# Attention ahead of two Strassen layers on one core: a pair's output split into an even part and an odd part with both tails, and the tail's copies moved to ScalarE

## The chip, the core and the metric

One core of a Trainium2 chip runs the whole program. The metric is the time of one execution on the device in microseconds, median of several runs. Engines: TensorE (PE: matmuls, their weight loads are PEld), VectorE (DVE), ScalarE (ACT), GpSimd (POOL) and SyncE (SP), which here issues all transfers.

## What is computed

```python
def _attn_ref(q, k, v):                 # q, k, v: (4, 8, 576, 64) fp32
    scores = scale * np.matmul(q, k.transpose(0, 1, 3, 2))
    rel = pos[:, None] - pos[None, :]
    bias = slopes[:, None, None] * (-np.abs(rel))[None, :, :]
    mask = (rel >= 0) & (rel < 128)
    scores = np.where(mask, scores + bias[None], -1000000000.0)
    scores = scores - np.max(scores, axis=-1, keepdims=True)
    attn = np.exp(scores)
    attn = attn / (np.sum(attn, axis=-1, keepdims=True) + 1e-09)
    return np.matmul(attn, v)

# then x = heads side by side: (2304, 512), and two layers:
h = x @ w_in                            # (512, 2048)
g = h * (1.0 / (1.0 + np.exp(-1.702 * h)))     # second layer: a clipped square instead
x = g @ w_out                           # (2048, 512)
```

## The kernel before, in words

The kernel has two stages. The first, attention, takes the first 160 us; the second, the two layers as Strassen-like products of split fp32 operands (`multiply`, line 1053), takes the rest. TensorE passes from one to the other in `duo` (line 1133), whose first call still holds the last pair's transposes.

**Attention.** 32 heads are handled as 16 pairs (an even head and an odd one). A head has 576 rows: four blocks of 128 and a tail of 64. A block of queries sees 256 keys. A pair is five steps (`ITEMS`, line 44): step 1 is block 0 of both heads, step 2 blocks 1 and 2 of the even head, step 3 block 3 of both, step 4 blocks 1 and 2 of the odd head, step 0 the tails of both heads in one bank. Their order in a pair is `STEP_ORDER` = 2, 3, 0, 1, 4 (in the first pair 2, 4, 3, 0, 1), so there are 80 steps, and every engine has a loop over m = 0 to 79 and some drain, written out by hand with lags. Write E for the last step of a pair. At m:

- TensorE (line 1164) makes the scores of step m (line 987), then values times probabilities for a group whose last step lies 4 or 5 steps back (`weigh_values`, lines 1015 and 1021), then transposes the probabilities of step m-2 (line 1000), then, at E+6, the four transposes of a pair's output (`transpose_pair`, line 1030) and at E+9 the one of its tail (`transpose_pair_tail`, line 1035). The tail's probabilities are a group with step 1.
- VectorE (line 1634): at E+5 first `write_pair` (line 1562: add 1e-9 to the sums, reciprocal, multiply), then the bias and the maximum of the scores of step m (line 1557; 1551 for the tails), then extra work: rounding of a head four heads on (line 1533, at E+1 and E+3 of the pair two before; called the cast), some sums and splits of weights and of the next stage's operands at single steps (m = 41, 46, 51, 61, 66, 71, 76), and at E+10 `copy_pair_tail` (line 1573, two copies of 64 x 64).
- ScalarE (line 1278): the copy of the transposed probabilities out of PSUM (line 1234), the exponentials of step m (line 1206; 1201 for the tails), and at E+7 `copy_pair` (line 1229).
- GpSimd (line 936): behind each cast the differences of keys and of queries (lines 889 and 893), and in between some work on weights (903, 913) and operands (929).
- SyncE: loads of heads and values, `store_pair` five pairs behind (line 592, waits for `pair_copied` and `pair_tail_copied`).

A pair's output has ten slots of 65 columns (64 and the sum), slot 2 * block + head; slots 0 to 4 are in PSUM bank 5 and 5 to 9 in bank 6. Three score banks, two for transposed probabilities (3 and 7) and one for transposed outputs (2) are the others. The semaphore `pair_written` is waited for by the next pair's first values (step 2) and by `transpose_pair`; `pair_tail_copied` by the next `transpose_pair`; `pair_copied` by `transpose_pair_tail`; `pair_tail_transposed` by the write after the next.

## Time and profile before

| | us |
|---|---|
| median of 3 runs | 870.99 (870.75 to 872.83) |
| the profiled execution, whole | 870.5 |
| its span, first to last instruction | 868.7 |
| granted clock of TensorE, mean | 0.998 of full |
| busy: TensorE / VectorE / ScalarE / GpSimd | 851.5 / 713.5 / 537.4 / 115.2 |

In rows with a time first, the columns are start and duration in microseconds, then engine, line of the kernel, instruction, and out<-in by the program's names; a bracket at the end is the time that the engine stood idle before it and whose end released it. Ends of matmuls are modelled, so that a row's duration can reach a little past the next row's start. In rows over stretches the granted clock (PEclk) is a share of full speed.

### The profile page before, as it was taken

The page shows a single profiled execution, that of the slowest core. Times are in us where ns is not written, and L with a number is a line of the kernel's source. Part 1 is how long each engine was busy: PE and PEld are TensorE (multiplying, and loading weights), DVE is VectorE, ACT ScalarE, POOL GpSimd, SP SyncE. Part 2 cuts the span into 40 slices and gives each one's busy share as a digit, 9 for nine tenths or more (in the row PEclk, how much of TensorE's full clock was granted, in tenths as well). Part 3 has the DMA queues.
Part 4 walks back from the last instruction along what each step waited for, and adds up shares of the span by engine and source line. Part 5 has one row for each costly group of instructions (what it writes and reads, how often), then busy time and mean ns, then how long its engine had stood idle before and what let it go on. Part 6 is the DMA issues. An engine that isn't in the chain of part 4 may idle for free.

```text
span 868.7 us, 15510 instructions
## 1 busy us (share of the span) xinstructions
PE 851.5 (98%) x5746; PEld 845.4 (97%) x5746; DVE 713.5 (82%) x984; ACT 537.4 (62%) x788; POOL 115.2 (13%) x81
## 2 busy tenths in 40 slices
PE   7999999999999999999999999999999999999998
PEld 7999889999999999999999999999999999999998
DVE  7889897577798868677997988898989779889784
ACT  5887778576774545676744555767556467765441
POOL 4787788000000000000000000000000000000000
PEclk9999999999999999999999999999999999999999
DMA  8876951568667265587775664488556643888822
GB/s 191 214 206 186 241 151 67 189 233 307 219 206 278 97 255 192 210 316 252 266 242 219 243 231 161 135 307 295 195 194 220 229 156 146 290 287 303 307 75 73
DMA packets 63241, 186.45 MB, mean 215 GB/s; under 512 B 7488, under 2 KB 14336, under 8 KB 59328
## 3 DMA queue, kind: packets, MB, share of 16 engines
q1 hardware_dynamic: 63168, 185.46, 63.0%
q8 instruction: 47, 0.77, 0.4%
q14 instruction: 26, 0.21, 0.1%
HBM read 113.09 MB, written 72.35 MB: 213 GB/s over the span
## 4 chain that ended last, share of the span: by engine, by line
PE 87%; DVE 6%; POOL 3%; issue 3%; ACT 1%; DVEq 0%; POOLq 0%; ACTq 0%
PE ps L1053 80%; PE ps L1021 3%; PE ps L987 2%; DVE qk_hi L1533 2%; PE ps L1000 1%; DVE probs L1557 1%; POOL qk_hi L893 1%; POOL k_lo L889 1%; DVE wst L1590 1%; PE ps L1030 0%; PE ps L1015 0%; DVE heads_out L1570 0%; DVE w_first L1603 0%; POOL qk_raw L933 0%; POOL wst L903 0%
## 5 line engine op out<-in xcount | busy, mean ns | idle before, releaser
L1053 PE MATMUL ps<-arena,w_first 128*128 128x384 f32 x1764 | 331.5, 336 | 0.9 <-ACT ps L1305 0.8
L1053 PEld LDWEIGHTS ps<-arena,w_first 128*128 128x128 f32 x1764 | 310.7, 188 | 2.4 <-issue 1.7
L1053 PE MATMUL ps<-arena,w_rest 128*128 128x384 f32 x1260 | 240.8, 337 | 0.9 <-ACT ps L1305 0.8
L1053 PEld LDWEIGHTS ps<-arena,w_rest 128*128 128x128 f32 x1260 | 220.1, 188 | 2.0 <-issue 1.7
L1661 DVE TENSOR_TENSOR arena<-raw_first,arena 128x768 fp32r<-128x768 f32 (+1 forms) x114 | 148.8, 1318 | 78.0 <-ACT arena L1272 78.0
L1272 ACT ACTIVATE arena<-raw_first 128x768 fp32r<-128x768 f32 (+1 forms) x120 | 132.0, 1117 | 45.6 <-DVE raw_first L1619 39.1
L1053 PE MATMUL ps<-w_rest,arena 128*128 128x256 f32 x945 | 132.4, 281 | 0.0
L1053 PEld LDWEIGHTS ps<-w_rest,arena 128*128 128x128 f32 x945 | 121.1, 189 | 0.1
L1053 PE MATMUL ps<-w_first,arena 128*128 128x256 f32 x567 | 88.0, 282 | 0.0
L1661 DVE TENSOR_TENSOR arena<-raw_rest,arena 128x1536 fp32r<-128x1536 f32 (+1 forms) x48 | 71.3, 1486 | 11.6 <-ACT arena L1272 11.5
L1053 PEld LDWEIGHTS ps<-w_first,arena 128*128 128x128 f32 x567 | 76.0, 189 | 0.0
L1272 ACT ACTIVATE arena<-raw_rest 128x1536 fp32r<-128x1536 f32 (+1 forms) x48 | 60.9, 1268 | 23.0 <-PE ps L1053 21.0
L1021 PE MATMUL ps<-v_sb,probs_t 128*128 128x65 f32 x448 | 58.0, 271 | 6.6 <-DVE heads_out L1570 6.6
L1206 ACT ACTIVATE probs<-probs,neg_max 128x256 f32<-128x256 f32 (+1 forms) x128 | 54.1, 472 | 15.3 <-DVE neg_max L1557 15.3
L1021 PEld LDWEIGHTS ps<-v_sb,probs_t 128*128 128x128 f32 x448 | 55.9, 193 | 7.9 <-issue 7.9
L1314 ACT ACTIVATE d1s<-ps 128x384 f32<-128x384 f32 (+2 forms) x72 | 35.3, 490 | 39.9 <-PE ps L1053 39.8
L1305 ACT ACTIVATE ps<-ps 128x384 f32<-128x384 f32 (+2 forms) x72 | 34.0, 475 | 31.0 <-PE ps L1053 31.0
L1590 DVE TENSOR_TENSOR wst<-wst 128x256 f32<-128x256 f32 (+1 forms) x93 | 50.5, 543 | 2.9
L1557 DVE CUSTOM_DVE_ANT_0 probs<-ps,bias_sb 128x256 f32<-128x256 f32 (+1 forms) x128 | 44.6, 385 | 8.7 <-PE ps L987 5.7
L987 PE MATMUL ps<-qk_hi 128*128 128x256 f32 x160 | 48.8, 327 | 1.6 <-POOL k_lo L875 1.4
L1234 ACT ACTIVATE probs_t<-ps 128x512 f32<-128x512 f32 x64 | 37.7, 590 | 16.2 <-PE ps L1000 15.7
L889 POOL TENSOR_TENSOR k_lo<-qk_raw,qk_hi 128x576 fp32r<-128x576 f32 x30 | 43.5, 1450 | 25.4 <-DVE qk_hi L1533 25.0
(116 smaller groups left out, 971.8 us busy)
## 6 DMA issues: line engine op xcount, KB each, us to landing
gd<-g SPq DMA_DIRECT2D x24, 1536.0 KB, 6.1
raw_rest<-gd SPq DMA_DIRECT2D x32, 768.0 KB, 5.1
wst<-w_pairs SPq DMA_DIRECT2D x32, 512.0 KB, 6.1
raw_first<-gd SPq DMA_DIRECT2D x16, 768.0 KB, 6.2
yd<-ust SPq DMA_DIRECT2D x6, 1536.0 KB, 6.3
qk_raw<-qkT SPq DMA_DIRECT2D x30, 288.0 KB, 4.4
wd<-ust SPq DMA_DIRECT2D x4, 1536.0 KB, 9.4
raw_first<-yd SPq DMA_DIRECT2D x4, 1536.0 KB, 7.8
```

The costliest lines, as they stand in the source:

```text
L889: nc.gpsimd.tensor_tensor(k_lo[:, slot], keys(qk_raw, head), f32(keys(qk_hi, head)), ALU.subtract).then_inc(qk_split[slot], 1)
L987: last = nc.tensor.matmul(place, queries, k[:, key0:key0 + BAND], start=n_pass == 0 and (d > 0 or i == 0), stop=n_pass == 1 and (d > 0 or ...
L1021: last = nc.tensor.matmul(o_slot(2 * blk + e), probs_t[:, gi % 2, col:col + P], v_sb[:, h + e, max(blk - 1, 0) + piece], start=piece == 0, ...
L1053: last = nc.tensor.matmul(to, stationary, moving, start=start and n == 0, stop=n == len(steps) - 1, skip_group_check=True)
L1206: last = nc.scalar.activation(at, at, ACT.Exp, bias=neg_max[:, col:col + 1], scale=-1.0)
L1234: nc.scalar.activation(probs_t[:, gi % 2], pt_bank[gi % 2], ACT.Copy).then_inc(pt_copied[gi % 2], 1)
L1272: nc.scalar.activation(operand(k, i)[:, 0], source(k, i), ACT.Copy).then_inc(hi_made, 1)
L1305: nc.scalar.activation(b_bank(D, pos), a_bank(D, pos), ACT.Copy).then_inc(seeded_b, 1)
L1314: nc.scalar.activation(d1(D, pos), d_bank(D, pos), ACT.Copy).then_inc(d_copied, 1)
L1557: last = nc.vector.tensor_tensor_reduce(out=to[:, 0:width], in0=bank[:, i * BAND:i * BAND + width], in1=bias_sb[:, h + e, BAND - width:BAN ...
L1590: nc.vector.tensor_tensor(to, a, b, ALU.subtract).then_inc(w_added, 1)
L1661: nc.vector.tensor_tensor(at[:, 1], source(k, i), f32(at[:, 0]), ALU.subtract).then_inc(lo_made, 1)
```

## The change

The ten slots are laid out anew: bank 5 holds blocks 0 to 3 of the even head, bank 6 blocks 0 to 3 of the odd head and then both tails. Each bank is a part with its own write, its own tile of inverses and its own semaphore. VectorE writes the even part at E+4 and the odd part at E+5, each behind the bias of that step (before: both at E+5, ahead of it). The next pair's values wait for the part that they overwrite: step 2 for the even part, step 3 for both. The pair's transposes come at E+7 (before E+6), its copy on ScalarE at E+8 (before E+7). The tail's transpose stays at E+9 and its copies at E+10, but the copies are ScalarE's, save the last pair's.

```diff
+OUT_SLOTS = (((0, 0), (0, 1), (0, 2), (0, 3)), ((1, 0), (1, 1), (1, 2), (1, 3), (0, 4), (1, 4)))
...
-WRITE_LAG = 5
-PAIR_LAG = 6
-COPY_LAG = 7
+WRITE_LAGS = (4, 5)
+PAIR_LAG = 7
+COPY_LAG = 8
 PAIR_TAIL_LAG = 9
 COPY_TAIL_LAG = 10
...
-    o_banks = ps[:, 5:7, 0:SLOTS // 2 * VALUES].rearrange("p b (s n) -> p b s n", n=VALUES)
+    o_banks = [ps[:, bank, 0:slots * VALUES].rearrange("p (s n) -> p s n", n=VALUES)
+               for bank, slots in zip((5, 6), map(len, OUT_SLOTS))]
...
+    def out_part(e, blk):
+        return int((e, blk) not in OUT_SLOTS[0])
+
+    def o_slot(e, blk, count=1):
+        part = out_part(e, blk)
+        slot = OUT_SLOTS[part].index((e, blk))
+        return o_banks[part][:, slot] if count == 1 else o_banks[part][:, slot:slot + count]
...
-                wait_past(pe, pair_written, q)
+            for part in range(2):
+                if any(out_part(e, blk) == part for e, blk in ITEMS[d]):
+                    wait_past(pe, written[part], q)
...
-                    nc.tensor.matmul(o_banks[:, 1, 3:5], probs_t[:, gi % 2, col:col + P],
+                    nc.tensor.matmul(o_slot(0, 4, 2), probs_t[:, gi % 2, col:col + P],
...
-                    last = nc.tensor.matmul(o_slot(2 * blk + e), probs_t[:, gi % 2, col:col + P],
+                    last = nc.tensor.matmul(o_slot(e, blk), probs_t[:, gi % 2, col:col + P],
...
         def transpose_pair(q):
-            pe.wait_ge(pair_written, q + 1)
+            for part in range(2):
+                pe.wait_ge(written[part], q + 1)
...
+        def copy_pair_tail(q):
+            pair = q % BATCH_PAIRS
+            act.wait_ge(pair_tail_transposed, q + 1)
+            for half in range(2):
+                rows = slice(half * TAIL, (half + 1) * TAIL)
+                last = nc.scalar.activation(x_pairs[rows, pair, 4 * P:SEQ], xt_bank[rows, rows], ACT.Copy)
+            last.then_inc(pair_tail_copied, 1)
...
-        for m in range(ALL_STEPS + TRANSPOSE_LAG):
+        for m in range(ALL_STEPS + DRAIN + 1):
...
             if (q := pair_at(m, COPY_LAG)) is not None:
                 copy_pair(q)
+            if (q := pair_at(m, COPY_TAIL_LAG)) is not None:
+                copy_pair_tail(q)
...
-        def write_pair(q):
-            at = inverse[:, q % SUM_RING]
-            dve.wait_ge(pv_done, 4 * (q + 1))
-            nc.vector.tensor_scalar(at, o_banks[:, :, :, DIM], 1e-9, None, ALU.add).then_inc(sums_guarded, 1)
...
+        def write_out(q, part):
+            at, bank = inverse[part][:, q % SUM_RING], o_banks[part]
+            to = heads_out[:, q % 2].rearrange("p (b e d) -> p b e d", e=2, d=DIM)
+            last = max(i for i, (pair, m) in enumerate(GROUPS)
+                       if pair == q and any(out_part(e, blk) == part for e, blk in ITEMS[ORDER[m][1]]))
+            dve.wait_ge(pv_done, last + 1)
+            nc.vector.tensor_scalar(at, bank[:, :, DIM], 1e-9, None, ALU.add).then_inc(sums_guarded, 1)
+            dve.wait_ge(sums_guarded, 2 * q + part + 1)
+            nc.vector.reciprocal(at, at).then_inc(sums_inverted, 1)
+            dve.wait_ge(sums_inverted, 2 * q + part + 1)
             wait_past(dve, pair_tail_transposed, q - 1)
...
+            last = nc.vector.tensor_tensor(to[:, 0:4, part], bank[:, 0:4, 0:DIM],
+                                           at[:, 0:4].unsqueeze(2).to_broadcast([P, 4, DIM]), ALU.mult)
+            if part:
+                last = nc.vector.tensor_tensor(to[:, 4], bank[:, 4:6, 0:DIM],
+                                               at[:, 4:6].unsqueeze(2).to_broadcast([P, 2, DIM]), ALU.mult)
+            last.then_inc(written[part], 1)
...
-            if (q := pair_at(m, WRITE_LAG)) is not None:
-                write_pair(q)
             if m < ALL_STEPS:
                 bias_scores(m)
+            for part in range(2):
+                if (q := pair_at(m, WRITE_LAGS[part])) is not None:
+                    write_out(q, part)
...
-            if (q := pair_at(m, COPY_TAIL_LAG)) is not None:
-                copy_pair_tail(q)
```

## Rows read from the trace of the kernel before

**Rows 1.** The page: busy time, and the chain that ended last, by line.
```profile
PE 851.5 (98%) x5746; PEld 845.4 (97%) x5746; DVE 713.5 (82%) x984; ACT 537.4 (62%) x788; POOL 115.2 (13%) x81
...
PE ps L1053 80%; PE ps L1021 3%; PE ps L987 2%; DVE qk_hi L1533 2%; PE ps L1000 1%; DVE probs L1557 1%; POOL qk_hi L893 1%; POOL k_lo L889 1%; DVE wst L1590 1%; PE ps L1030 0%; PE ps L1015 0%; DVE heads_out L1570 0%; DVE w_first L1603 0%; POOL qk_raw L933 0%; POOL wst L903 0%
```

**Rows 2.** Stretches: length, busy PE, PEld, DVE, ACT, POOL, clock, DMA share, GB/s.
```profile
40.00:60.00 20.00, 20.00 (x183) 20.00 (x182) 17.15 (x65) 15.27 (x37) 16.30 (x12) 1.00 0.75 196
...
120.00:140.00 20.00, 16.95 (x150) 16.61 (x151) 19.77 (x57) 14.18 (x30) 16.49 (x11) 1.00 0.36 101
```

**Rows 3.** Timeline of VectorE, line 1570: four writes of a pair.
```profile
31.40 0.82 DVE L1570 TENSOR_TENSOR heads_out<-ps,inverse 128x640 f32<-128x640 f32 x1
39.46 0.82 DVE L1570 TENSOR_TENSOR heads_out<-ps,inverse 128x640 f32<-128x640 f32 x1
...
72.08 0.82 DVE L1570 TENSOR_TENSOR heads_out<-ps,inverse 128x640 f32<-128x640 f32 x1
...
81.89 0.82 DVE L1570 TENSOR_TENSOR heads_out<-ps,inverse 128x640 f32<-128x640 f32 x1
```

**Rows 4.** Waits, 0 to 170 us: total, times, longest.
```profile
PE ps L1021 <- DVE heads_out L1570: 6.6, 7, 1.5
```

**Rows 5.** Timeline, 74 to 85 us: casts on VectorE, GpSimd's operations beside them.
```profile
74.40 1.83 POOL L913 TENSOR_TENSOR w_first<-wst,w_first 128x768 fp32r<-128x768 f32 x1
...
74.71 2.14 DVE L1533 CAST qk_hi<-qk_raw 128x1152 fp32r<-128x1152 f32 x1
...
78.48 2.01 POOL L893 TENSOR_TENSOR qk_hi<-qk_raw,qk_hi 64x576 fp32r<-64x576 f32 x1
...
79.41 1.69 DVE L1533 CAST qk_hi<-qk_raw 128x1152 fp32r<-128x1152 f32 x1
...
84.99 0.76 DVE L1533 CAST qk_hi<-qk_raw 128x1152 fp32r<-128x1152 f32 x1 [0.41 <-DMA qk_raw<-qkT]
```

**Rows 6.** Timeline of VectorE around the write at 81.89.
```profile
81.24 0.28 DVE L1557 CUSTOM_DVE_ANT_0 probs<-ps,bias_sb 128x128 f32<-128x128 f32 x1
...
81.45 0.15 DVE L1565 TENSOR_SCALAR inverse<-ps 128x10 f32<-128x10 f32 x1
81.64 0.22 DVE L1567 RECIPROCAL inverse<-inverse 128x10 f32<-128x10 f32 x1
...
82.63 0.41 DVE L1557 CUSTOM_DVE_ANT_0 probs<-ps,bias_sb 128x256 f32<-128x256 f32 x1
...
83.31 0.45 DVE L1578 COPY x_pairs<-ps 64x64 f32<-64x64 f32 x2
```

**Rows 7.** The chain that ended last, in order of time, near 50 us: start, length.
```profile
50.25 1.30 DVE qk_hi L1533
```

**Rows 8.** Timeline of TensorE: values behind the wait for a write.
```profile
101.41 1.08 PE L1021 MATMUL ps<-v_sb,probs_t 128*128 128x65 f32 x8 [0.97 <-DVE heads_out L1570]
...
147.57 1.08 PE L1021 MATMUL ps<-v_sb,probs_t 128*128 128x65 f32 x8 [0.21 <-DVE heads_out L1570]
```

**Rows 9.** Timeline at the end of attention, 154 to 157 us.
```profile
154.70 0.17 DVE L1565 TENSOR_SCALAR inverse<-ps 128x10 f32<-128x10 f32 x1 [5.12 <-PE ps L1021]
...
154.84 1.22 PE L1053 MATMUL ps<-arena,w_first 128*128 128x384 f32 x6
...
156.48 0.63 PE L1030 MATMUL ps<-ident,heads_out 128*128 128x128 f32 x4 [0.42 <-DVE x_pairs L1578]
```

**Rows 10.** ScalarE's copies from 30 to 130 us: busy, mean ns, idle before.
```profile
L1229 ACT ACTIVATE x_pairs<-ps 128x512 f32<-128x512 f32 x12 | 7.0, 582 | 0.0
...
L1256 ACT ACTIVATE w_first<-wst 128x256 fp32r<-128x256 f32 x2 | 0.8, 409 | 0.0
```

**Rows 11.** Timeline, 46 to 48 us: exponentials of a tail, then a tail's transpose.
```profile
46.24 0.46 ACT L1201 ACTIVATE probs_tail<-probs_tail,neg_max 128x192 f32<-128x192 f32 x1
...
47.32 0.27 PE L1035 MATMUL ps<-ident,heads_out 128*128 128x128 f32 x1
```

**Rows 12.** Stretches around the low clock, columns as in rows 2.
```profile
98.00:102.00 4.00, 2.61 (x22) 2.23 (x21) 3.93 (x16) 2.83 (x5) 2.54 (x3) 1.00 0.40 105
102.00:106.00 4.00, 4.00 (x24) 4.00 (x24) 2.86 (x11) 2.31 (x6) 3.08 (x4) 0.57 1.03 296
```

More of the change, by code:

```diff
@@ L151, in build @@
     neg_max = sb("neg_max", [P, 2 * (STEPS - 1) + TAIL_RING], F32, attn_ctx)
-    inverse = sb("inverse", [P, SUM_RING, 2, SLOTS // 2], F32, attn_ctx)
+    inverse = [sb(f"inverse{part}", [P, SUM_RING, len(OUT_SLOTS[part])], F32, attn_ctx) for part in range(2)]
     probs_t = sb("probs_t", [P, 2, 4 * P], F32, attn_ctx)
@@ L194, in build @@
     sums_inverted = sem("sums_inverted")
-    pair_written = sem("pair_written")
+    written = [sem("first_part_written"), sem("second_part_written")]
     pair_transposed = sem("pair_transposed")
@@ L317, in all_queries @@
         return tile[rows, head % SPLIT_RING, at:at + SEQ]
-    def o_slot(slot):
-        return o_banks[:, slot // (SLOTS // 2), slot % (SLOTS // 2)]
+    def out_part(e, blk):
[4 more added lines that the diff above has]
+        return o_banks[part][:, slot] if count == 1 else o_banks[part][:, slot:slot + count]
     def up_duo(u, c, dd):
@@ L1560, in bias_scores, with copy_last_tail @@
             last.then_inc(scores_biased, 1)
-        def write_pair(q):
-            at = inverse[:, q % SUM_RING]
-            dve.wait_ge(pv_done, 4 * (q + 1))
-            nc.vector.tensor_scalar(at, o_banks[:, :, :, DIM], 1e-9, None, ALU.add).then_inc(sums_guarded, 1)
-            dve.wait_ge(sums_guarded, q + 1)
+        def write_out(q, part):
[6 more added lines that the diff above has]
+            dve.wait_ge(sums_guarded, 2 * q + part + 1)
             nc.vector.reciprocal(at, at).then_inc(sums_inverted, 1)
-            dve.wait_ge(sums_inverted, q + 1)
+            dve.wait_ge(sums_inverted, 2 * q + part + 1)
             wait_past(dve, pair_tail_transposed, q - 1)
-            nc.vector.tensor_tensor(heads_out[:, q % 2].rearrange("p (b s d) -> p b s d", b=2, d=DIM), o_banks[:, :, :, 0:DIM],
-                                    at.unsqueeze(3).to_broadcast([P, 2, SLOTS // 2, DIM]), ALU.mult).then_inc(pair_written, 1)
-        def copy_pair_tail(q):
-            pair = q % BATCH_PAIRS
-            dve.wait_ge(pair_tail_transposed, q + 1)
+            last = nc.vector.tensor_tensor(to[:, 0:4, part], bank[:, 0:4, 0:DIM],
[4 more added lines that the diff above has]
+            last.then_inc(written[part], 1)
+        def copy_last_tail():
+            dve.wait_ge(pair_tail_transposed, PAIR_COUNT)
             for half in range(2):
                 rows = slice(half * TAIL, (half + 1) * TAIL)
-                last = nc.vector.tensor_copy(x_pairs[rows, pair, 4 * P:SEQ], xt_bank[rows, rows])
+                last = nc.vector.tensor_copy(x_pairs[rows, BATCH_PAIRS - 1, 4 * P:SEQ], xt_bank[rows, rows])
             last.then_inc(pair_tail_copied, 1)
@@ L1633, in _ @@
         round_first(0)
-        for m in range(ALL_STEPS + COPY_TAIL_LAG - 1):
-            if (q := pair_at(m, WRITE_LAG)) is not None:
-                write_pair(q)
+        for m in range(ALL_STEPS + WRITE_LAGS[1]):
             if m < ALL_STEPS:
                 bias_scores(m)
+            for part in range(2):
+                if (q := pair_at(m, WRITE_LAGS[part])) is not None:
+                    write_out(q, part)
             if m == 0:
@@ L1779, in up @@
                 if k == 0:
-                    copy_pair_tail(PAIR_COUNT - 1)
+                    copy_last_tail()
                 add_weights(w + (3 if u < 2 else 4))
```

## The prediction

> **What bounds the kernel now.** I read the page first: TensorE is busy 98% of the span, and line 1053, the product stage, makes up 80% of the chain that ended last [rows 1]. The diff touches only the attention stage, the first 160 us. So the question is how much earlier attention can end; from there on TensorE runs without a gap, and what attention saves the whole keeps.
>
> Inside attention the stretches come next [rows 2]. From 40 to 60 us TensorE is busy throughout and VectorE 17.15 of 20; from 120 to 140 VectorE is busy 19.77 and TensorE 16.95. The engine that sets the pace changes. The starts of the write of a pair show the same [rows 3]: 8.06 us from 31.40 to 39.46, but 9.81 from 72.08 to the next write at 81.89 [rows 3]. Of the fifteen distances between the sixteen writes four are slow like this one; a fifth slow one has another cause, below. The waits then name what the change aims at: TensorE waits 6.6 us in seven places for the write of a pair (L1570 before L1021) [rows 4]. That 6.6 is the naive gain.
>
> It isn't the gain that I expect, since waiting is where TensorE's slack shows in a slow pair, not what makes it slow. VectorE's own rows in the pair before 81.89 have no gap: a cast of 2.14 us at 74.71, then an extra operation on weights, then a cast of 1.69 at 79.41 [rows 5]. Casts take 0.76 where GpSimd is quiet (84.99). The long ones end about 0.6 us after GpSimd's operation beside them: 74.40 + 1.83 = 76.23 against 76.85, and 78.48 + 2.01 = 80.49 against 81.10 [rows 5]. GpSimd in turn waits for the cast. The slow pair is thus a loop of cast, GpSimd, extra operation, cast; the write lies behind the second cast and outside the loop. The Trainium skill (SBUF — State Buffer, "SBUF: two separate sides") says that VectorE in a two-port mode and GpSimd exclude each other for a whole instruction; by that rule the cast's length is a wait that swallows work put ahead of it. These rows agree. By the rule VectorE's extra work there (0.10 a pair, below) costs nothing; by the bare durations it would cost 0.5 over five pairs.
>
> **The change, part by part.**
>
> Work on VectorE. A pair costs it now, from start to start: sum 0.19 (81.45 to 81.64), reciprocal 0.25 (to 81.89), multiply 0.74 (from 81.89 to 82.63) [rows 3, 6], and two tail copies, 0.45 busy together [rows 6], 0.48 with the hand-over: 1.66. After: sum and reciprocal twice, 0.88 (their small widths matter little: I keep the price for 10 columns), and multiplies of 256, 256 and 128 columns. The 640-column one takes 0.74 to the next start. If its columns cost 1.04 ns each, as 0.82 busy less a fixed 0.15 (the 10-column sum's whole duration) says, it has 0.67 of columns and 0.07 fixed, so 0.34 + 0.34 + 0.20 = 0.88. Sum 1.76, or 0.10 more a pair; between 0 (narrow sums are cheaper) and 0.3 (each of four extra instructions costs its own 0.15 without overlap, less the copies). In the loop above it is hidden by GpSimd; in fast pairs by VectorE's gaps of 1.2 to 1.7 us. It shows only where GpSimd is back to back, in the 16 us of the chain behind the cast at 50.25 [rows 7]. That cast starts after both parts instead of after write and copies: later by about 0.15. **Cost 0.15.**
>
> The earlier release. The next pair's first values (step 2) now need only the first part, which is behind one score operation and 0.78 us of writing instead of 1.18: 0.40 sooner, so I take 0.46 with the shorter end of the multiply. But step 3 needs the second part: 0.78 + 0.76 (bias of the next step: 0.68 from 82.63 to 83.31, and hand-over) + 0.98 + 0.1 of hand-over = 2.6 after the last short bias (begun at 81.24, over at 81.45) [rows 6], that is 84.1; TensorE's own path, led by 0.46, gets there at about 84.1 too. Net lead 0.36, between 0.2 and 0.46. It counts only where a slow pair is followed by a TensorE-bound one: from the values at 101.41 on, and again a pair before 147.57 [rows 8]. **Gain 0.72.** In other slow pairs the wait only moves. At 147.57 TensorE waits 0.21 by the row [rows 8]; modelled ends run some 0.16 past the next start, so really about 0.37. Even part written by then: **gain 0.37.**
>
> The end. At 156.48 the last pair's transposes waited (0.42 by the row) for the tail copy of the pair before, queued behind the last write; the product ahead of them began at 154.84 and needs 1.22 less the modelled 0.16, to 155.90 [rows 9]. Now ScalarE copies that tail from about 154.8, where its queue is empty, and the last odd part is ready at 154.70 + 0.19 + 0.25 + 0.34 + 0.25 + 0.1 = 155.83, before the transposes can start at 155.95. **Gain 0.53** (between 0.3 and 0.6).
>
> Tail copies on ScalarE. No row shows it copying 64 columns. Below: half of VectorE's 0.45 for two [rows 6]; above: its own 256-column copy of 0.41. I take 0.28 each, by 0.58 for 512 columns and the slope between those two [rows 10]. The Trainium skill (VectorE: DVE Perf Modes, "The TRN2 errata") gives ScalarE 172 + columns cycles from PSUM, which would be an estimate of 0.20; nothing would change. About 0.5 a pair, where ScalarE is busy 15.27 of 20 us [rows 2]: hidden. The transposes of a pair (lag 7) need this copy (lag 10 of the pair before, the same step less two): it ends about 42.4, they run at about 43.8. Slack 1.4.
>
> The pair copy one step later (lag 8). It now comes after the tail's exponentials at 46.24 and starts 0.36 behind them, at 46.60, ending 47.18; TensorE loads the tail's transpose 0.11 before 47.32 [rows 11]. With 0.05 of hand-over it is late by about 0.04 where it had slack of over a microsecond. Eight TensorE-bound pairs: **cost 0.30**, bounds 0 and 1.6 (0.2 each). In slow pairs this wait is larger (the copy would end near 80.6, the tail's transpose was due at about 79.9), but TensorE has 1.5 us to spare there and merely waits earlier.
>
> SyncE stores a pair five pairs later than the one being loaded; that leaves a tail about 10 us. No DMA is added or moved, and half a microsecond more on a tail doesn't reach its queue.
>
> Sum: 0.72 + 0.37 + 0.53 - 0.15 - 0.30 = **1.17 gained** against the profiled execution's 870.5. The runs' median is 870.99, so I forecast 869.8.
>
> **Rivals.** (A) *The clock stays up.* The granted clock is 0.57 on average from 102 to 106, once in attention [rows 12]: mostly the lower level, 1.2 of 2.4 GHz. It follows four microseconds in which TensorE was busy 2.61. Lost: 4 x 0.43 = 1.7, which makes the fifth slow pair. In the other slow pairs the idle is one block and the clock held. After the change much idle moves ahead of the tail's transpose, as one block of some 1.6. For: the idle is short and can go either way. Against: the busy total of four microseconds hardly changes. 869.8 - 1.7 = 868.1.
> (B) *The waits were the bound*: all 6.6 and the 0.42 at the end go, and the clock's 1.7: 871.0 - 8.7 = 862.3. Against it is VectorE without a gap.
> (C) *Slower: the pair copy.* If ScalarE reaches it later than worked out (the exponentials of the tail, weights rounded and tail copies in the same queue), the tail's transpose holds every score behind it. At 0.3 us in each of 16 pairs it costs 4.8 in place of 0.3: 874.3. It decides from (2.6 + 1.17 + 0.3) / 16 = 0.25 a pair. For it: the slack I work out is nothing. Against: ScalarE has idle stretches in every pair.
> (D) *VectorE's additions count*: the casts don't absorb them in the five slow pairs (0.5), and the lead of 0.72 is lost: 869.8 + 1.2 = 871.0. The ends of the casts speak against.
>
> **How the numbers follow.** Forecast 0.38, A 0.30, B 0.08, C 0.10, D 0.14. A measurement can tell about 0.3% from no change, 2.6 us. Faster than 868.4: A lies 0.3 beyond that line, so most of it, and all of B, with a part of the forecast's own scatter, 0.32. Slower than 873.6: C and a little more, 0.10. Within: 0.58. The range leaves out B and C: from 867.2 (A with costs at 0 and gains at their upper ends is 867.4, and runs scatter by some tenths) to 871.6 (D, with the pair copy at 0.11 a pair).
>
> **What would show it.** Right: VectorE's rows without a gap and write-to-write distances near 9.8 in the same slow pairs; the wait of L1021 for a write well under 6.6, with a new wait of TensorE at the tail's transpose (L1035) for ScalarE's pair copy in its place; the last pair's transposes directly behind the product. Wrong: slow pairs near 8.1 (B), a wait at L1035 in pairs that took 8.06 (C), or 8.06 itself changed. A low clock anywhere in attention tells A from the forecast.

## The result, and the profile after

The changed kernel takes **872.4 us**, median of 20 runs (871.99 to 874.97), beside 870.92 of the kernel before, also 20 runs (870.5 to 872.83). The ratio is 1.0015, 95% interval 1.0009 to 1.0021: slower by 1.5 us, less than 0.2% but clear of no change, where the prediction had 1.17 us of gain and a range that ended at 871.6. The profiled execution took 872.12 us, its span 870.3.

First the page of the changed kernel: busy time, and the chain that ended last, by line. The product stage is now line 1066, the scores 997, the values 1033, the transposes of a pair 1043, the cast 1556, GpSimd's two differences 899 and 903.

```profile
PE 853.2 (98%) x5746; PEld 843.8 (97%) x5746; DVE 713.7 (82%) x1018; ACT 544.9 (63%) x818; POOL 114.3 (13%) x81
...
PE ps L1066 80%; PE ps L1033 3%; PE ps L997 2%; PE ps L1010 2%; DVE qk_hi L1556 2%; POOL qk_hi L903 2%; POOL k_lo L899 1%; DMA qk_raw<-qkT 1%; PE ps L1043 1%; DVE probs L1580 1%; PE ps L1027 1%; DVE wst L1620 0%; ACT w_first L1280 0%; SPq L583 0%; SPq L582 0%
```

The totals hardly move against [rows 1]: VectorE has 0.2 us more. The busy totals don't tell where 1.5 us went. One name is new in the chain: a load of heads (DMA qk_raw<-qkT, 1%), which [rows 1] doesn't have. The same stretches as in [rows 2] and [rows 12] (length, busy PE, PEld, DVE, ACT, POOL, clock, DMA share, GB/s) tell more:

```profile
40.00:60.00 20.00, 19.64 (x173) 19.01 (x172) 16.68 (x69) 15.95 (x40) 15.63 (x12) 1.00 0.73 198
...
120.00:140.00 20.00, 17.90 (x151) 16.59 (x150) 19.73 (x61) 15.50 (x36) 16.38 (x11) 1.00 0.38 101
...
98.00:102.00 4.00, 3.10 (x29) 2.86 (x27) 3.96 (x8) 2.20 (x5) 2.63 (x2) 1.00 0.79 199
102.00:106.00 4.00, 3.52 (x29) 3.28 (x30) 3.64 (x20) 3.96 (x10) 3.56 (x3) 1.00 0.54 166
```

From 40 to 60 us TensorE, which had no gap before, starts 173 matmul instructions instead of 183: the pairs that TensorE used to pace are now slower. And the clock stays at its upper level, 2.4 GHz, from 102 to 106. Rival A's condition came true, and the time still rose.

The start of the tail's transpose (L1035 before, L1048 after) marks each pair. The distances between these sixteen starts, in us, worked out from the timelines:

```
          first at  pairs up to 82             then one, four, one, one  last two   last at
before      31.19   8.05 8.08 8.08 8.07 8.40 8.05   9.78 | 8.67 11.50 8.05 8.81 | 9.84 9.81 | 8.12 5.02   159.52
after       31.66   8.11 8.51 8.31 8.50 8.51 8.50   9.47 | 10.73 8.56 8.51 9.82 | 9.83 9.48 | 7.76 4.80   161.06
difference  +0.47   +1.71 in all                   -0.31 | +0.59 in all         | -0.01 -0.33 | -0.36 -0.22  +1.54
```

The sum, 1.54, is the whole loss. The largest part is 1.71 in the six pairs that TensorE used to pace: four now take 8.50 instead of 8.05 to 8.40. The +0.47 at the start is not read further: over all kernels of this document that first start lies anywhere from 30.9 to 31.8. The middle four hold, before, the low clock; more on that below.

The load lies just ahead of the distance of 10.73. In the chain of waits (start, length) it releases the cast of an even head at 87.28:

```profile
81.71 5.54 DMA qk_raw<-qkT
```

The waits of the changed kernel from 0 to 172 us (total, times, longest):

```profile
POOL k_lo L899 <- DVE qk_hi L1556: 28.0, 27, 2.5
...
PE ps L997 <- POOL qk_hi L903: 3.2, 9, 0.5
...
PE ps L1033 <- DVE heads_out L1597: 1.9, 5, 0.4
PE ps L1048 <- ACT x_pairs L1242: 1.7, 4, 1.2
```

TensorE's wait for a write fell from 6.6 [rows 4] to 1.9, as the change meant it to. But 3.2 us of waiting for GpSimd and 1.7 for ScalarE's pair copy stand there now: 6.8 in all, so the waits have changed their name. And the same view of the kernel before gives GpSimd less idleness:

```profile
POOL k_lo L889 <- DVE qk_hi L1533: 25.0, 25, 1.9
```

GpSimd waits 3 us longer for casts after the change. The chain of waits of the changed kernel, in order of time (start, length), shows where GpSimd stands in the path. It is one full turn of a pair, in the fourth of the six distances, from the scores at 53.24 to those at 61.74, and the turn is 8.50 us long:

```profile
53.24 0.49 PE ps L997 x4
...
53.93 0.11 DVE probs_tail L1574
...
54.30 1.90 DVE qk_hi L1556
...
56.33 1.43 POOL k_lo L899
...
57.83 1.41 POOL qk_hi L903
...
59.29 0.74 PE ps L997 x4
60.03 0.84 PE ps L1033 x8
60.86 0.44 PE ps L1010 x4
61.31 0.44 PE ps L1043 x4
61.74 0.47 PE ps L997 x4
```

Read it as a loop: scores of the tails (step E+8, which is E+3 of the next pair), their bias, the cast of the odd head, GpSimd's two differences, and then the scores of E+7, which need the head just split, with their values and transposes, until the scores of E+8 again. Of this turn GpSimd's stretch is fixed. What TensorE does between the scores of E+7 and those of E+8 is not covered by anything. The change has put the four transposes of the pair there (L1043, 0.44). Not every slow turn is this loop: in the fifth distance the chain runs from 63.52 to 67.45 through ScalarE's queue, its copy of the pair (0.39) among it.

A second part is in VectorE. This is its timeline in the changed kernel, from the bias of E+5 to the casts, with GpSimd's operations beside them:

```profile
48.28 0.27 PE L1048 MATMUL ps<-ident,heads_out 128*128 128x128 f32 x1
...
49.26 0.43 DVE L1580 CUSTOM_DVE_ANT_0 probs<-ps,bias_sb 128x256 f32<-128x256 f32 x1 [0.62 <-PE ps L1010]
...
50.10 0.16 DVE L1592 TENSOR_SCALAR inverse<-ps 128x6 f32<-128x6 f32 x1
...
51.05 0.41 DVE L1580 CUSTOM_DVE_ANT_0 probs<-ps,bias_sb 128x256 f32<-128x256 f32 x1
...
51.74 0.77 DVE L1556 CAST qk_hi<-qk_raw 128x1152 fp32r<-128x1152 f32 x1
...
52.65 1.42 POOL L899 TENSOR_TENSOR k_lo<-qk_raw,qk_hi 128x576 fp32r<-128x576 f32 x1 [0.76 <-DVE qk_hi L1556]
...
54.15 1.42 POOL L903 TENSOR_TENSOR qk_hi<-qk_raw,qk_hi 64x576 fp32r<-64x576 f32 x1
...
54.22 1.97 DVE L1556 CAST qk_hi<-qk_raw 128x1152 fp32r<-128x1152 f32 x1
```

The odd cast, 1.97 us long, ends at 56.19, 0.62 behind the end of GpSimd's operation at 54.15 + 1.42 = 55.57, as the long casts of [rows 5] did. Before, the whole write stood ahead of the bias of E+5 and began while VectorE still waited for these scores, so it was free; behind the bias only the tail's copies stood (0.48). After, the odd part stands behind that bias: 50.10 to 51.05, 0.95. From the tail's transpose to the even cast it was 50.17 - 47.32 = 2.85 before and is 51.74 - 48.28 = 3.46 here; in all six pairs the cast starts 0.45 to 0.6 later than it did.

Whether GpSimd then starts later is another question, and in this pair it doesn't. These are the same two operations in the kernel before:

```profile
50.17 1.38 DVE L1533 CAST qk_hi<-qk_raw 128x1152 fp32r<-128x1152 f32 x1
...
51.69 1.42 POOL L889 TENSOR_TENSOR k_lo<-qk_raw,qk_hi 128x576 fp32r<-128x576 f32 x1 [0.76 <-DVE qk_hi L1533]
```

The cast came earlier but ran longer, until 51.55, 0.62 behind the end of GpSimd's work on weights (50.93), and GpSimd's difference began 51.69 - 47.32 = 4.37 behind the tail's transpose; after, 52.65 - 48.28 = 4.37. The timelines of the other pairs show that the late cast reaches GpSimd only in the first two of the six (4.16 against 3.71 in both); in the last four GpSimd's work on weights covers it. What is late in the pair shown is the odd cast, by 0.24, because the values of E+7 wait for the odd part (1.04 in the chain for 0.84) and the tails' scores come behind them. TensorE waits for GpSimd where the late cast reaches it, at 42.46, and again at 59.29:

```profile
42.46 0.39 PE L997 MATMUL ps<-qk_hi 128*128 128x256 f32 x1 [0.17 <-POOL qk_hi L903]
...
59.29 0.39 PE L997 MATMUL ps<-qk_hi 128*128 128x256 f32 x1 [0.19 <-POOL qk_hi L903]
...
61.50 0.37 PE L997 MATMUL ps<-qk_hi 128*128 128x256 f32 x1
```

At the same place before, GpSimd's operation ended at 56.62 + 1.41 = 58.03, just ahead of the scores that need it at 58.10, and from these to the next scores it was 1.77 us against 61.50 - 59.29 = 2.21:

```profile
57.75 0.60 PE L1030 MATMUL ps<-ident,heads_out 128*128 128x128 f32 x4
...
58.10 0.37 PE L987 MATMUL ps<-qk_hi 128*128 128x256 f32 x1
...
59.87 0.37 PE L987 MATMUL ps<-qk_hi 128*128 128x256 f32 x1
```

From this came two theories, which can both hold: **late transposes** (L in the expectations below: the pair's transposes at E+7 lie in the uncovered part of the loop) and **late cast** (W: the odd part stands ahead of the even cast, and GpSimd starts late). Their rivals were the prediction's C (ScalarE's pair copy at the tail's transpose) and D (VectorE's additional work by its mere amount).

### The profile page after: what moved, and what is told of

Its sections match the earlier page's. It is cut to its first block, busy times and chain, and to the rows that moved or that the text cites. A ratio compares the mean times of both kernels' runs of the same rounds, so it can differ in the third digit from the quotient of the medians.

```text
span 870.3 us, 15634 instructions
## 1 busy us (share of the span) xinstructions
PE 853.2 (98%) x5746; PEld 843.8 (97%) x5746; DVE 713.7 (82%) x1018; ACT 544.9 (63%) x818; POOL 114.3 (13%) x81
## 4 chain that ended last, share of the span: by engine, by line
PE 88%; DVE 4%; POOL 3%; issue 2%; DMA 1%; ACT 1%; SPq 1%; DVEq 0%; POOLq 0%; ACTq 0%
PE ps L1066 80%; PE ps L1033 3%; PE ps L997 2%; PE ps L1010 2%; DVE qk_hi L1556 2%; POOL qk_hi L903 2%; POOL k_lo L899 1%; DMA qk_raw<-qkT 1%; PE ps L1043 1%; DVE probs L1580 1%; PE ps L1027 1%; DVE wst L1620 0%; ACT w_first L1280 0%; SPq L583 0%; SPq L582 0%
## 5 line engine op out<-in xcount | busy, mean ns | idle before, releaser
L1328 ACT ACTIVATE ps<-ps 128x384 f32<-128x384 f32 (+2 forms) x72 | 34.0, 475 | 28.8 <-PE ps L1066 28.8
```

The source lines that it names most:

```text
L1328: nc.scalar.activation(b_bank(D, pos), a_bank(D, pos), ACT.Copy).then_inc(seeded_b, 1)
```

## The experiments

Thirteen kernels ran. Each ratio is against the kernel before, on the same chip. "After" and "before" in front of an edit say which kernel it was made in.

**e1_pair8** (after): the pair's transposes one step later still, out of that part of the loop.

```diff
-PAIR_LAG = 7
+PAIR_LAG = 8
```

> The changed kernel with the pair's transposes one step later still (lag 8 instead of 7). Theory L (loop): in the fast pairs the scores of the odd head (step E+7) wait for GpSimd's split of that head, which follows the cast behind the tail's bias (scores of E+3); the change put the pair's transposes (0.44 us) between the scores of E+7 and those of E+8, the one stretch of that loop in which GpSimd has nothing to do. At lag 8 they lie under GpSimd's work again: fast pairs go back from 8.50 to about 8.1, some 2.2 us less up to 82 us, whole time 869 to 870.3. Rival W (VectorE): the second write in front of the even cast makes the loop long by itself; the distances stay at 8.5 and the time at 872.4. Rival C (ScalarE's pair copy at the tail's transpose): stays at 872.4 or gets worse, since the copy is closer to the tail's transpose.

Measured: 871.84, ratio 1.0005 [0.9996, 1.0014], above what was expected. The 0.5 us that it gains is no larger than the uncertainty of the two medians. Its first distances are 8.12 8.22 8.31 8.21 8.69 8.41, not 8.06, so something else holds the loop as well.

**e2_before_pair7** (before): only the transposes and their copy one step later, with one whole write as before.

```diff
-PAIR_LAG = 6
-COPY_LAG = 7
+PAIR_LAG = 7
+COPY_LAG = 8
...
-        for m in range(ALL_STEPS + TRANSPOSE_LAG):
+        for m in range(ALL_STEPS + TRANSPOSE_LAG + 1):
```

> The kernel before with only the pair's transposes one step later (lags 7 and 8 for 6 and 7). Theory L by itself: up to 0.44 us more in each TensorE-bound pair, less where GpSimd's split is done early (from 44.65 to 49.54 in the trace of before, 0.5 ahead of its scores): between 871 and 873.5. If theory W holds alone, no change: 870.9. Theory C (copy one step later behind the tail's exponentials): waits at the tail's transpose in the fast pairs, 0.04 to 0.3 each.

Measured: 871.7, ratio 1.0010 [1.0001, 1.0019], 0.8 us slower. Its distances are 8.06 8.11 8.06 8.51 8.52 8.48, then 9.48 9.85 8.57 8.48 9.82 9.82 9.5, 8.1, 5.03. The fourth to sixth are those of the changed kernel to 0.02, so the 8.50 there comes from this move alone. The first three are not (8.06 8.11 8.06 against 8.11 8.51 8.31): these 0.7 us, and more in the middle (9.85 against 10.73), belong to the rest of the change. The run moves ScalarE's copy of the pair together with the transposes, and doesn't tell the two apart. Ahead of the 9.85 the load is shorter: 5.2 us from its issue to the cast that waits for it, against 6.1 in the changed kernel, and that cast starts 1.4 us earlier. It has the wait of the tail's transpose for ScalarE's pair copy too, in five places against four (here and in the experiments below, fences of this form are waits from 0 to 172 us):

```profile
PE ps L1021 <- DVE heads_out L1570: 3.6, 5, 0.8
...
PE ps L1035 <- ACT x_pairs L1229: 1.8, 5, 1.2
```

**e3_pair6** (after): transposes and copy where they were before.

```diff
-PAIR_LAG = 7
-COPY_LAG = 8
+PAIR_LAG = 6
+COPY_LAG = 7
```

> The changed kernel with the transposes back at lag 6 and the copy at 7. They then need the odd part, which VectorE finishes about 0.6 us after TensorE gets there. Theory L: the wait takes the place of the 0.44, fast pairs 8.5 to 8.7, time 872 to 873.5, and no wait of the scores for GpSimd. Theory C: the pair copy is early again, so 870 to 871.

Measured: 875.39, ratio 1.0054 [1.0041, 1.0067]. Far slower, for a reason that I hadn't expected. The transposes don't wait for the odd part but for ScalarE's copies of the tail of the pair before, in 14 pairs:

```profile
PE ps L1043 <- ACT x_pairs L1249: 10.7, 14, 1.2
```

The first eight distances are 8.87 to 9.08. So the transposes *had* to move once the copies had become ScalarE's.

**f3_before_act_tails** (before): nothing but the tail's copies moved to ScalarE (`copy_pair_tail` as in the diff, at E+10 behind `copy_pair`), to ask that directly.

> The kernel before with only the tails' copies moved to ScalarE (all but the last pair's), lags as they were. The transposes of the next pair at E+6 then wait for a copy that stands behind the exponentials of E+5 (with lag 6 in the changed kernel that wait was 10.7 us in 14 places, 0.6 to 1.2 each). Expected: waits of 0.5 to 0.7 in each pair, fast pairs 8.6 to 8.9, 873 to 876. If ScalarE's copies are hidden as the prediction had it, 870.5.

Measured: 874.14, ratio 1.0036 [1.0023, 1.0048], with the same wait:

```profile
PE ps L1030 <- ACT x_pairs L1236: 9.4, 14, 0.8
```

The copies themselves are short, but ScalarE reaches them too late for transposes at E+6.

**f4_dve_tails** (after): the tail's copies back on VectorE, behind the odd part (`copy_last_tail(q)` at COPY_TAIL_LAG for every pair).

> The changed kernel with the tails' copies back on VectorE behind its other work of the step (two parts and lag 7 stay). Theories L and W: 0.48 us more in front of the even cast in each pair, so the loop over GpSimd is longer still: fast pairs 8.6 to 9.0, 873.5 to 876, and the last pair's transposes wait again for the copy. If VectorE's work in front of the cast is free: 872.4.

Measured: 873.22, ratio 1.0027 [1.0018, 1.0036], 0.8 slower than the changed kernel, with intervals that just touch. The six fast distances are 0.7 longer in all, and GpSimd's first difference starts later in each of them, by 0.26 to 0.49. This is the direct measure of what 0.48 us more ahead of the even cast costs. With the new write order ScalarE's copies do pay; they take 0.48 out of what lies between bias and cast.

**e4_half_split** (after): GpSimd's difference for the queries made for 288 columns of 576. This leaves out the low part of half of the queries.

```diff
-                nc.gpsimd.tensor_tensor(all_queries(qk_hi, head, LOWER), all_queries(qk_raw, head, UPPER),
-                                        f32(all_queries(qk_hi, head, UPPER)), ALU.subtract).then_inc(qk_split[slot], 1)
+                nc.gpsimd.tensor_tensor(all_queries(qk_hi, head, LOWER)[:, 0:SEQ // 2], all_queries(qk_raw, head, UPPER)[:, 0:SEQ // 2],
+                                        f32(all_queries(qk_hi, head, UPPER)[:, 0:SEQ // 2]), ALU.subtract).then_inc(qk_split[slot], 1)
```

> The changed kernel with GpSimd's difference of the queries made for 288 of the 576 columns only (left out: the low part of half of the queries of most heads). Each such operation is about 0.7 us shorter. Theories L and W, both of which need GpSimd in the chain: fast pairs back to 8.1, slow pairs shorter by 1 or more, time 866 to 869. Theory C or a chain of TensorE, VectorE and ScalarE alone: fast pairs stay at 8.5.

Measured: 863.34, ratio 0.9912 [0.9898, 0.9926]. Nine microseconds go, more than expected, and the first six distances are 8.11 to 8.33. The two rows are groups of instructions from 30 to 130 us (busy, mean ns | idle before), the first of the changed kernel, the second of this one:

```profile
L903 POOL TENSOR_TENSOR qk_hi<-qk_raw,qk_hi 64x576 fp32r<-64x576 f32 x23 | 35.1, 1526 | 1.8
```

```profile
L903 POOL TENSOR_TENSOR qk_hi<-qk_raw,qk_hi 64x288 fp32r<-64x288 f32 x24 | 21.9, 913 | 1.9
```

0.61 us less per head, 1.2 per pair. The slow pairs fall from 9.5 to 9.8 to between 8.2 and 9.0, and TensorE's wait for GpSimd's queries is gone from the list. VectorE has the same instructions in this kernel, but its casts are shorter as well, 1.045 us in the mean against 1.344, since they end behind GpSimd's operations. This puts GpSimd into the path. It speaks against D, though VectorE's busy time fell too, so it doesn't exclude it.

**g1_cast1** (after): the even cast one step earlier, so that it stands ahead of the odd part.

```diff
-CAST_LAG = (2, 3)
+CAST_LAG = (1, 3)
```

> The changed kernel with the even head's cast one step earlier, transposes at lag 7 as in the change. With the runs so far (changed 872.4, lag 8 alone 871.8, lag 8 and early cast 870.2) this closes the square. If the two effects add, 872.4 - 1.6 = 870.8. If the place of the transposes costs 0.44 by itself whenever GpSimd's second split ends late, fast pairs stay at 8.3 to 8.5 in part: 871 to 872. If only the cast's lateness mattered: 870.2, as with lag 8.

Measured: 870.58, ratio 0.9994 [0.9985, 1.0003]. The second distance is back at 8.12, the first six together are 50.36 against 50.44, and the sixth alone is longer, 9.05.

**f1_pair8_cast1** (after): both, `PAIR_LAG = 8` and `CAST_LAG = (1, 3)`.

> The changed kernel with the pair's transposes at lag 8 and the cast of the even head one step earlier on VectorE (lag 1 for 2), so ahead of the bias of step E+6. In the first run with lag 8 the fast pairs took 8.2 to 8.7, not 8.06. Theory W (the second write in front of the even cast makes GpSimd's split of the even head end late, and the odd cast wait for it): the cast ahead gives that back, fast pairs 8.06 to 8.1, no wait of the scores for GpSimd before 80 us; 870.5 or less, against 871.8 with lag 8 alone. If the lateness of the even cast does not matter, 871.8 again.

Measured: 870.18, ratio 0.9992 [0.9983, 1.0001]. With e1 and g1 this is a square, of medians with intervals about 0.8 us to each side:

```
                         transposes at E+7     at E+8
even cast at lag 2            872.4 (after)      871.8 (e1)
even cast at lag 1            870.6 (g1)         870.2 (f1)
```

In time alone, the early cast gives 1.7 (1.8 and 1.6 with either place of the transposes), clear of the intervals; the transposes' place gives 0.5 (0.6 and 0.4), which isn't. But the 1.7 is what a whole step earlier gives, and not what the change's half microsecond had cost. The fast pairs gain next to nothing (f1: 8.12 8.11 8.31 8.22 8.42 9.04, where 8.06 to 8.1 was expected); from the seventh tail's transpose to the last it is 78.96 in the changed kernel and 77.75 in g1, so the gain lies in the slow pairs. The load that the cast at 87 waits for also differs: from issue to cast 6.1 us in the changed kernel, 6.6 in e1, 6.5 in g1 and 5.4 in f1, one execution of each, so part of the difference between e1 and f1 may be its scatter.

**f2_before_cast1** (before): `CAST_LAG = (1, 3)` alone, to see if it is simply a better place.

> The kernel before with only the cast of the even head one step earlier. Theory: GpSimd's idle time ahead of its splits (25.0 us before) falls wherever it sets the pace, so the slow pairs shorten or the stretch behind 48 us loses its 0.4; 869.5 to 870.9. The rival, that VectorE's total alone counts: 870.9.

Measured: 882.94, ratio 1.0135 [1.0121, 1.0149]. Twelve microseconds slower: in the old order the cast came to stand ahead of the tail's copies, for which the transposes wait:

```profile
PE ps L1030 <- DVE x_pairs L1578: 14.3, 13, 2.0
```

**g2_before_cast1_copy** (before): the same, with the tail's copies moved ahead of the cast.

```diff
-CAST_LAG = (2, 3)
+CAST_LAG = (1, 3)
...
+            if (q := pair_at(m, COPY_TAIL_LAG)) is not None:
+                copy_pair_tail(q)
...
-            if (q := pair_at(m, COPY_TAIL_LAG)) is not None:
-                copy_pair_tail(q)
```

> The kernel before with the even cast one step earlier but behind the tail's copies (in the run with the cast ahead of them TensorE waited 13.9 us for those copies, 882.9). Theory: fast pairs are TensorE's own 8.06 and stay; slow pairs, which are the loop of cast and GpSimd, get GpSimd's start some 0.7 earlier and shorten from 9.8 towards 9.1: 868.5 to 870. The rival, that in the slow pairs VectorE's busy time is the bound: 870.9.

Measured: 867.39, ratio 0.9961 [0.9949, 0.9974]: faster than both kernels by 3.5 and 5.0 us. The waits show what happened, 7 us less for GpSimd than before:

```profile
POOL k_lo L889 <- DVE qk_hi L1533: 18.0, 18, 1.9
...
PE ps L1021 <- DVE heads_out L1570: 3.7, 5, 1.4
```

The wait that the change set out to remove falls by 2.9 without touching the write, because slow pairs are fewer and shorter (9.65 8.58 9.07 8.08 8.95 9.68 9.11). The 9.07 stands where the low clock made 11.50 in the trace of before, but the clock isn't the gain: seven executions of the kernel before on this chip kept the upper level throughout (granted clock 1.0), and their median is 870.95. So the same step earlier gives 3.5 in a kernel in which nothing had made the cast late. Here the chain of waits in the stretch from 48 to 66 us holds TensorE alone, a turn of 8.07 from one set of transposes to the next:

```profile
49.59 0.44 PE ps L1030 x4
...
57.66 0.44 PE ps L1030 x4
```

**g3_pair8_cast12** (after): both casts a step earlier.

```diff
-PAIR_LAG = 7
+PAIR_LAG = 8
...
-CAST_LAG = (2, 3)
+CAST_LAG = (1, 2)
```

> The changed kernel with lag 8 and both heads' casts one step earlier. Theory: the odd cast then stands ahead of the tail's bias, finds GpSimd still in the even head's split and holds VectorE's queue until it ends (up to 2 us), so the tail's exponentials and the pair copy behind them come late: new waits of TensorE at the tail's transpose or the tail's probabilities, 871 to 876. If only GpSimd's start mattered: below 870.2.

Measured: 870.84, ratio 0.9999 [0.9990, 1.0008]: nothing won over f1. Distances reach 9.96, with waits of the tail's transpose for ScalarE's pair copy of 0.8 to 1.05 us in six places, as expected.

**h1_best_end** (g2, and ScalarE copies the tail of pair 14 alone): the one gain that the changed kernel showed clearly, taken without the rest.

```diff
+        act.wait_ge(pair_tail_transposed, PAIR_COUNT - 1)
+        for side in range(2):
+            rows = slice(side * TAIL, (side + 1) * TAIL)
+            last = nc.scalar.activation(x_pairs[rows, BATCH_PAIRS - 2, 4 * P:SEQ], xt_bank[rows, rows], ACT.Copy)
+        last.then_inc(pair_tail_copied, 1)
...
+            if (q := pair_at(m, COPY_TAIL_LAG)) is not None and q < PAIR_COUNT - 2:
+                copy_pair_tail(q)
```

> The kernel before with the even cast early, behind the tail's copies (867.4), and of the change only the end: the tail of the last pair but one is copied by ScalarE. The prediction priced the end at 0.53. In the kernel before, the last pair's transposes waited 0.42 for this copy; without that wait the distance between the last two transposes of a tail falls from 5.03 to between 4.5 and 4.8, and the time to 866.9 to 867.2.

Measured: 866.84, ratio 0.9954 [0.9939, 0.9969]. The last distance is 4.80 instead of 5.03. Its median is 0.55 below g2's, with intervals too wide to prove that from the time alone; against the kernels before and after it is faster, by 4.1 and 5.6 us.

**h2_no_tail_multiply** (f1 without the tails' multiply; the tails' rows of the output are set to zero once, at the start): is the length of the odd part still in the path?

```diff
-            if part:
-                last = nc.vector.tensor_tensor(to[:, 4], bank[:, 4:6, 0:DIM],
-                                               at[:, 4:6].unsqueeze(2).to_broadcast([P, 2, DIM]), ALU.mult)
```

> The changed kernel with lag 8 and early even cast, without the multiply of the two tails (left out: the tails' rows of the attention output are zeros), so that the odd part is written 0.2 to 0.3 us sooner. Theory V: in the fast pairs the values of step E+7 wait some 0.15 to 0.25 for the odd part, hidden behind the modelled ends; fast pairs go from 8.1 to 8.4 down to 8.06 to 8.15. If the odd part is not what is late: unchanged, 8.2 to 8.4.

Measured: 868.98, ratio 0.9979 [0.9970, 0.9988], 1.2 below f1. The first three distances go from 8.12 8.11 8.31 to 8.06 8.05 8.16, and only 0.3 of the 1.2 lies in the first six. So its length still counts a little. In the changed kernel the values behind the scores at 51.04 need the odd part, which is over at 50.86 + 0.28 = 51.14, and start at 51.28, where the order of TensorE alone would have let them start at about 51.16 (the values of the other steps start 0.12 behind the last score instruction). That is a third price of the split, some 0.1 per fast pair and 0.25 in the third distance, which stays at 8.3 in the changed kernel, e1, g1 and f1 alike and is 8.06 in e2; the next distances (8.24, 8.42) don't follow it.

## Why the prediction was wrong

Step by step, as the prediction put it.

**What bounds the kernel: right, but kept to the slow pairs.** The loop of cast and GpSimd was described for the slow pairs and left out of the fast ones, which the prediction took to be TensorE's. They were TensorE's by a hair: GpSimd ended at 58.03 and TensorE needed it at 58.10. The chain of waits had said it ([rows 7] lies in a chain that runs through GpSimd for 16 us): two engines were both in the path in the fast pairs.

**The transposes' move: the step that failed.** The prediction put it at nothing, without a reason: it asks whether the transposes find their inputs at E+7 and not what they push back. They push the scores of E+8 back by 0.44 where GpSimd covers nothing. Moved by themselves (with ScalarE's copy of the pair) they make the kernel before 0.8 us slower (e2, between 0.1 and 1.7), and three of the six fast distances of the changed kernel are those of e2.

**"Cost 0.15": too low, and from the wrong comparison.** It compared VectorE's total of a pair before and after, 1.66 and 1.76. The total was good: sum, reciprocal and multiplies take 0.95 for the odd part (50.10 to 51.05) and 0.74 for the even one (56.53 to 57.27), 1.69. But what counts is how much of it stands behind the scores of E+5 and ahead of the even cast, and that went from 0.48 to 0.95, since the write of before stood in an idle stretch of VectorE. The cast is later by about 0.46, not by 0.15, in every fast pair. That GpSimd hides this, as the prediction said, is right for four of the six; in the other two it goes through, and g1, with the cast a step earlier, gives the second distance back (8.51 to 8.12). With the wait for the odd part it makes the 0.7 us by which the first three distances are longer than in e2.

**Earlier release, gain 0.72 and 0.37: half right.** The distance in which the values at 147.57 [rows 8] lie fell by 0.36 (8.12 to 7.76), as forecast, and e2 without the early release keeps 8.10 there. The two leads of 0.36 before it aren't seen. Two slow distances did fall, by 0.31 and 0.33, but e2 shows the same 9.48 and 9.5 with one whole write, so they belong to the moved transposes.

**The end, gain 0.53: right in mechanism, half of it kept.** From tail's transpose to the last transposes it was 156.48 - 154.50 = 1.98 [rows 9], and is 157.67 - 156.26 = 1.41:

```profile
156.26 0.28 PE L1048 MATMUL ps<-ident,heads_out 128*128 128x128 f32 x1
...
156.58 0.45 ACT L1249 ACTIVATE x_pairs<-ps 64x64 f32<-64x64 f32 x2 [0.92 <-PE ps L1048]
156.61 1.22 PE L1066 MATMUL ps<-arena,w_first 128*128 128x384 f32 x6
...
157.67 0.60 PE L1043 MATMUL ps<-ident,heads_out 128*128 128x128 f32 x4
...
157.93 0.86 ACT L1328 ACTIVATE ps<-ps 128x384 f32<-128x384 f32 x2 [0.90 <-PE ps L1066]
...
161.06 0.27 PE L1048 MATMUL ps<-ident,heads_out 128*128 128x128 f32 x1
```

0.57 is won. Then the second product takes longer, 161.06 - 157.67 = 3.39 against 159.52 - 156.48 = 3.04. ScalarE's operation on PSUM ahead of it (L1328) still has to wait for the first product, and TensorE, no longer held by a transpose, arrives earlier at what that operation frees; this is read from the rows and was not tested. Net 0.22, and 0.23 in h1, which has this part alone. What is next in line after the wait was removed, the prediction didn't ask here.

**Tail copies hidden on ScalarE: right, by the moved transposes alone.** After the move TensorE never waits for them. Without it they cost 3.2 us (f3). By f4 it also saves 0.8 us that VectorE no longer has them. The length of 0.28 each was too high: 0.211, see below.

**Pair copy at lag 8, cost 0.30: too high.** By the prediction's own terms it is 47.18 + 0.05 - 47.21 = 0.02 late and not 0.04, so even the sum was too high. Of the four waits for it (1.7 us in all) one, 0.18 at 82.10, closes a fast distance; the others, 1.2, 0.17 and 0.18, lie in slow pairs, where the prediction had said that TensorE merely waits earlier; the chain passes the 1.2 by, through the cast and GpSimd. In the fifth fast distance the copy does lie in the chain, in ScalarE's queue and not at the tail's transpose, and no run moves the copy alone. Rival C, whose sign came true, is not the mechanism: at its 0.3 in each of 16 pairs it would wait 4.8 us, four waits of 1.7 are there, and e2 has them too.

**Rival A: condition met, price not seen.** The clock stayed at its upper level throughout attention. The granted clock of single executions of the changed kernel is 1.0 in nine and 0.998 in six, and the two sorts have medians of 872.5 and 872.4 (one execution at 0.996 took 874.97). The kernel before, over the 79 executions beside the experiments, has medians of 870.84 at 1.0 (25 of them) and 870.84 at 0.996 (16). So a low stretch of this length does not show in the whole. The four middle distances of the ledger say the same: 37.03 with it in the kernel before, 37.62 without in the changed one, and 36.72 without in e2. The prediction's 1.7 for it is not borne out; what it costs exactly, no run tells.

**"Doesn't reach its queue": right for the stores only.** SyncE's load of heads at 81 us stands behind a load of weights that VectorE releases, so it starts 1.6 us later than before (81.20 against 79.62), and the cast that waits for it starts at 87.28 in place of 84.99. The prediction has no term for loads.

**Sum.** From the kernel before to e2 the last tail's transpose moves by +0.70 (159.52 to 160.22), and from e2 to the changed kernel by another +0.84. The second part is made up of -0.17 at the start, +0.70 in the first three distances, +0.88 in the eighth, and -0.34 and -0.23 for the release before the last pair and the end. In these terms the transposes' move and the split of the write cost about 0.7 each. The +0.88 is carried from the load, which takes 0.9 us longer than in e2; over ten traces it takes 5.2 to 6.6 us from issue to cast, and whether the change makes it long or these single executions scatter is open. So is why the slow distances fall by 0.3 in e2.

## What to carry to other kernels

When work is split or moved on an engine that feeds a loop over several engines, its total doesn't say what it costs; ask for each piece what it stands behind and ahead of, whether it has left an idle stretch for a place ahead of the operation that starts the slowest partner, and whether that partner was waiting for it there. Ask the same of whatever else moves to make room: here the four transposes, which nobody had counted. A wait that one engine shows in some turns is not the bound: look for the engine that ends within a tenth of a microsecond of being needed in the other turns, because the smallest delay there shows in full. Once such a loop is found, moving the start of its longest part earlier (here one cast by one step, with the copies kept ahead of it) was worth more than the wait that had drawn the eye. But the gain of an additional move is not the price of the first one, even when the numbers seem to add up; only the turns in which each shows can tell.

## What the runs showed of the hardware that I hadn't expected

ScalarE's copy of 64 columns out of PSUM takes 0.211 us, below the 0.28 taken and even the lower bound of 0.22 (groups of the changed kernel, 30 to 130 us: busy, mean ns | idle):

```profile
L1249 ACT ACTIVATE x_pairs<-ps 64x64 f32<-64x64 f32 x22 | 4.6, 211 | 0.1
```

The slope was too flat because its two rows are not of one kind: the 256-column copy (L1256) reads `wst` in SBUF, the 512-column one (L1229) reads PSUM. From ScalarE's operations on PSUM alone, 0.473 us for 384 columns and 0.796 for 768 (L1325 of the kernel before), 64 columns come out as 0.20. The estimate of 0.20 by the Trainium skill's figure (VectorE: DVE Perf Modes, "The TRN2 errata") is near as well; the trace agrees within 0.02.

Small multiplies on VectorE follow each other faster than their busy time says. The 256-column one has a mean of 0.425 busy, and the next starts 0.35 after it (50.51 to 50.86); the 128-column one has 0.280 busy and leaves 0.19 to the next start. The prediction's 0.34 and 0.20 from start to start hold:

```profile
L1597 DVE TENSOR_TENSOR heads_out<-ps,inverse 128x256 f32<-128x256 f32 x22 | 9.3, 425 | 0.8
...
L1600 DVE TENSOR_TENSOR heads_out<-ps,inverse 128x128 f32<-128x128 f32 x11 | 3.1, 280 | 0.0
```

And one step of order on one engine moves this kernel by more than the whole change did: the same cast, one step earlier in the kernel before, gives 882.9 ahead of the tail's copies and 867.4 behind them.
